# Banded attention in narrow query tiles: 32 local or 54 strided queries by 64 keys, stacked in the partitions, both heads in one transpose

## What is computed

```python
# 1: attention; heads 0-3 local, heads 4-7 strided
mask_local   = (rel >= 0) & (rel < 32)              # rel = query - key
mask_strided = (rel >= 0) & (key % 32 == query % 32)
attn = softmax(where(mask, q @ k.T / 8, -1e9)) @ v
# 2: x = attn (heads side by side, 512 wide)
theta = x @ w_theta
y = w_tok_r @ (x * cos(theta)) + w_tok_i @ (x * sin(theta))
u = x + y
x = u + relu(u @ w_ch)
# 3: four causal attention experts over x, top 2 of 4 by a gate, summed
```

## Time and profile before

| | us |
|---|---|
| median of 3 runs (584.88 to 585.02) | 584.98 |
| profiled execution, its own time | 586.84 |
| its span in the trace | 585.0 |
| TensorE matmul busy | 548.8 (94%) |
| VectorE busy | 348.0 (59%) |
| ScalarE busy | 259.3 (44%) |
| GpSimd busy | 130.4 (22%) |

### The profile page before, as it was taken

How to read it: one execution, slowest core, us unless ns; L and a number is a source line. 1 busy time by engine, 2 the same in 40 slices (tenths; PEclk the granted TensorE clock), 3 DMA queues, 4 the chain that set the end, 5 groups by cost and what they waited for, 6 DMA issues and landing times.

```text
span 585.0 us, 11660 instructions
## 1 busy us (share of the span) xinstructions
PE 548.8 (94%) x4473; PEld 468.8 (80%) x4473; DVE 348.0 (59%) x831; ACT 259.3 (44%) x774; POOL 130.4 (22%) x131
## 2 busy tenths in 40 slices
PE   6999999999999999999999999999999999998786
PEld 5777889989766799898866799898876799996555
DVE  1677856676779513676788622576778723344561
ACT  2774743556435531545533551455543551114242
POOL 3650800021312250013221250012322060000110
PEclk9999999999999999999999999999999999999879
DMA  9732046310000115121000014221000010000002
GB/s 219 198 92 74 1 126 152 77 29 21 2 1 2 72 23 120 41 55 28 3 0 2 37 47 113 62 46 31 8 2 1 34 49 1 1 1 1 1 0 82
DMA packets 73413, 27.13 MB, mean 46 GB/s; under 512 B 68624, under 2 KB 68624, under 8 KB 73360
## 3 DMA queue, kind: packets, MB, share of 16 engines
q1 hardware_dynamic: 68848, 24.38, 16.4%
q10 hardware_dynamic: 4512, 2.02, 1.4%
HBM read 21.67 MB, written 4.72 MB: 45 GB/s over the span
## 4 chain that ended last, share of the span: by engine, by line
PE 73%; DVE 15%; ACT 7%; issue 3%; POOL 1%; DVEq 0%; POOLq 0%; ACTq 0%
PE acc L1248 32%; PE wide L1248 14%; PE turned L1417 4%; PE wide L1320 4%; PE wide L1341 3%; PE turned L1361 3%; PE turned L1374 3%; DVE xt L1080 2%; PE turned L1391 2%; PE turned L1459 2%; ACT probs L877 2%; PE turned L1281 2%; DVE probs L1054 1%; DVE nmax L1023 1%; PE wide L1305 1%
## 5 line engine op out<-in xcount | busy, mean ns | idle before, releaser
L789 POOL TENSOR_TENSOR probs<-probs,rec 96x768 f32<-96x768 f32 (+1 forms) x16 | 21.7, 1354 | 203.1 <-DVE rec L1038 203.1
L870 ACT ACTIVATE probs<-wide,nmax 96x128 f32<-96x128 f32 (+1 forms) x176 | 61.3, 368 | 8.9 <-DVE nmax L1019 8.8
L885 ACT ACTIVATE pt<-turned 128x384 f32<-128x384 f32 (+3 forms) x64 | 30.8, 480 | 72.9 <-PE turned L1374 36.7
L877 ACT ACTIVATE probs<-wide,nmax 128x128 f32<-128x128 f32 (+4 forms) x72 | 39.0, 551 | 52.2 <-DVE nmax L1023 41.5
L798 POOL TENSOR_TENSOR probs<-probs,weight 128x128 f32<-128x128 f32 (+4 forms) x36 | 26.9, 767 | 155.6 <-DVE weight L1061 155.6
L1248 PE MATMUL wide<-w_tok_hi,z_hi 128*128 128x288 f32 x216 | 47.4, 300 | 0.0
L1248 PE MATMUL wide<-w_tok_hi,z_lo 128*128 128x288 f32 x216 | 46.0, 293 | 0.0
L1248 PE MATMUL wide<-w_tok_lo,z_hi 128*128 128x288 f32 x216 | 45.9, 293 | 0.0
L1023 DVE TENSOR_REDUCE nmax<-wide 128x1 f32<-128x128 f32 (+4 forms) x72 | 32.8, 512 | 16.9 <-PE wide L1346 16.9
L1248 PE MATMUL acc<-xu_hi,w_ch_hi 128*128 128x288 f32 x128 | 39.2, 306 | 2.0 <-DVE xu_lo L1150 2.0
L815 POOL TENSOR_TENSOR z_lo<-absf,z_hi 128x512 fp32r<-128x512 f32 x20 | 26.4, 1319 | 63.8 <-ACT z_hi L933 63.8
(11 more groups left out here) (190 smaller groups left out, 1479.5 us busy)
## 6 DMA issues: line engine op xcount, KB each, us to landing
raw_q<-in_q SPq DMA_DIRECT2D x32, 128.0 KB, 2.4
out<-o_sb SPq DMA_DIRECT2D x16, 256.0 KB, 2.0
raw_k<-in_k SPq DMA_DIRECT2D x28, 128.0 KB, 2.5
raw_v<-in_v SPq DMA_DIRECT2D x64, 31.5 KB
raw_v<-in_v SPq DMA_DIRECT2D x14, 120.0 KB
raw_r<-in_moe_w_tok_r SPq DMA_DIRECT2D x1, 1152.0 KB, 6.2
stage<-in_moe_w_theta ACTq DMA_DIRECT2D x2, 512.0 KB, 9.0
raw_i<-in_moe_w_tok_i SPq DMA_DIRECT2D x1, 1024.0 KB, 7.9
```

Of the source, the lines that this page charges most:

```text
L789: g.tensor_tensor(pr, pr, rec[0:rows, 1, 0:nt].unsqueeze(2).broadcast_to([rows, nt, w]), ALU.mult).then_inc(s["probs_pool"], 1)
L870: e = a.activation(probs[0:rows, hh, t * P:t * P + w], wide[slot][0:rows, t * P:t * P + w], ACT.Exp, bias=nmax[0:rows, hh, t:t + 1], accum ...
L877: e = a.activation(probs[:, hh, to0:to0 + n], wide[slot][:, at0:at0 + n], ACT.Exp, bias=nmax[:, hh, j:j + 1], accum_out=sums[:, hh, j:j + 1])
L885: ins = a.activation(dst, src, ACT.Copy)
```

## The change

The first attention gets smaller tiles, and several of them share a column of PSUM:

- A local tile is 32 queries by 64 keys (the 32 before and the tile's own 32), 18 per head. Four tiles stand above each other in the partitions, so a head has 5 columns of 64. A strided tile is 3 residues, 54 queries by 54 keys, 11 per head, two above each other, 6 columns.
- Both heads share one `wide` place, one bank each. The mask of a head is now one bf16 matmul (`copies_l` or `copies_s` by `mask_l` or `mask_s`), 320 or 384 wide, in place of three or two. One more small one per head (`never`) masks the keys before the first tile.
- The probabilities of the two heads lie side by side in `tiled` (head 0 in 64 columns, head 1 in the next 64), so one transpose turns both. `turn` is one step with 5 or 6 transposes in place of 12 or 10, and two copies in place of four. It waits for both heads: for VectorE's and for GpSimd's `norm`.
- `values` has one matmul for each small tile and head: 36 of 32 columns in place of 12 of 96, or 22 in place of 10. Its stationary operand is v, 64 columns wide as before, and head 1's rows are now 64 to 127.
- `max` reads 320 or 384 columns in place of 768 or 630, `exp` is 5 or 6 instructions per head of 64 columns in place of 6 or 5 of 128 or 126, and `norm` multiplies 320 or 384 columns.
- Order: between units of the first attention the scores come first and the whole turn after them. Before the third layer's first scores the whole turn comes first. In `LAST_PAIR` the turn comes behind three blocks of token weight transposes.
- Loads of v: a local pair's two heads lie in two halves of the partitions with the rows of v twice (6 DMAs as before, with 2304 rows of 256 bytes in place of 1472). A strided pair has 6 DMAs in place of 10.
- The constants are built in another order; the masks have a semaphore of their own (`masks`).

```diff
+W = 64
+L_T = S // STRIDE
+R_T = W // R_N
+COLS = (S_T * W + P - 1) // P
@@ attention_steps
+        if ahead and ahead[0] == "s1":
+            steps.append(("scores",) + ahead)
         if behind:
-            steps.append(("turn",) + behind + (0,))
+            steps.append(("turn",) + behind)
+        if ahead and ahead[0] != "s1":
+            steps.append(("scores",) + ahead)
         if ahead:
-            steps += [("scores",) + ahead, ("max",) + ahead + (0,)]
-        if behind:
-            steps.append(("turn",) + behind + (1,))
-        if ahead:
-            steps += [("max",) + ahead + (1,), ("exp",) + ahead + (0,)]
+            steps += [("max",) + ahead + (0,), ("max",) + ahead + (1,), ("exp",) + ahead + (0,)]
@@ LAST_PAIR
-LAST_PAIR = [("wtok", 0, "acc"), ("turn",) + S1_UNITS[-1] + (0,), ("wtok", NT, "wide"), ("wtok", 1, "wide"),
-             ("done", "wtok", 0, "acc"),
-             ("turn",) + S1_UNITS[-1] + (1,), ("values",) + S1_UNITS[-1], ("weights", 2),
+LAST_PAIR = [("wtok", 0, "acc"), ("wtok", NT, "wide"), ("wtok", 1, "wide"), ("done", "wtok", 0, "acc"),
+             ("turn",) + S1_UNITS[-1], ("values",) + S1_UNITS[-1], ("weights", 2),
@@ scores
+                    for hh in range(2):
+                        mm(wide[slot][:, hh * 512:hh * 512 + cols * W], copies[:, :],
+                           mask[:, :].unsqueeze(1).broadcast_to([part, cols, W]), start=True, stop=True,
+                           skip_group_check=True)
...
+                        row, at0 = part * t % P, part * t // P * W + (STRIDE if local(p) and t == 0 else 0)
+                        for hh in range(2):
                             hd = slice(hh * D, (hh + 1) * D)
+                            ins = mm(wide[slot][row:row + n, hh * 512 + at0:hh * 512 + at0 + q0 + n - k0],
+                                     qt[hd, q0:q0 + n], kt[hd, k0:q0 + n], start=False, stop=True,
+                                     skip_group_check=True)
@@ turn
+                            if n == 0:
+                                pe.wait_ge(s["probs_dve"], c.at("probs_dve"))
+                                pe.wait_ge(s["probs_pool"], c.at("probs_pool"))
+                            for t in range(ca, cb):
+                                k = min(P, part * nt - t * P)
+                                ins = nc.tensor.transpose(turned[slot][:, (t - ca) * P:(t - ca) * P + k],
+                                                          tiled[0:k, t, :], ident[0:k, 0:k])
@@ values
+                                ins = mm(turned[slot][hh * D:(hh + 1) * D, (t - ta) * rows:(t - ta) * rows + n],
+                                         raw_v[hh * W:hh * W + keys, p % 2, t, :],
+                                         tiled_t[hh * W:hh * W + keys, part * t:part * t + n], start=True, stop=True)
```

More of the change, by code:

```diff
@@ L178, in alone_steps @@
         nxt = units[i + 1] if i + 1 < len(units) else None
+        steps += early[i] + [("scores",) + ahead]
         if behind:
[L180 to L184, removed]
+            steps.append(("turn",) + behind)
+        steps += [("max",) + ahead + (0,), ("max",) + ahead + (1,), ("exp",) + ahead + (0,)]
         steps.append(("warm", 1 if nxt else 2, "acc", 1))
@@ L296, in psum_uses @@
     if k == "scores":
-        return ["wide"] * 2
+        return ["wide"] * (1 if step[1] == "s1" else 2)
     if k == "theta":
@@ L324, in events @@
         return {"negmax": 1}
+    if k == "exp" and step[1] == "s1" and step[4] == 0:
+        return {"exp_first": 1}
     if k == "norm":
@@ L533, in turned_copies @@
         def turned_copies(step, n, uses):
-            place, hh = turned[uses[n][0]], step[4]
+            place = turned[uses[n][0]]
             if step[1] == "s1":
-                rows, nt, w = tiles(step[2])
-                lo, hi = ((0, 3), (3, nt))[n]
-                return [(pt[0:w, hh, lo * rows:hi * rows], place[0:w, 0:(hi - lo) * rows])]
+                part, nt, _, cols = tiles(step[2])
+                lo, hi = ((0, 3 * P), (3 * P, nt * part))[n]
+                return [(tiled_t[:, lo:hi], place[:, 0:hi - lo])]
+            hh = step[4]
             blocks = turned_blocks(step[2], n, len(uses))
@@ L743, in after @@
                 step_n[0] += 1
[L745 removed]
+            for t, x in ((ident, 0.0), (ident_b, 0.0), (copies_l, 0.0), (copies_s, 0.0), (mask_l, 0.0), (mask_c, 0.0),
+                         (before, 0.0)):
                 after(g.memset(t[:], x))
+            after(g.memset(mask_s[:, 0:SQ], 0.0))
+            after(g.memset(mask_s[:, SQ:W], MASKED))
+            after(g.memset(never[:], MASKED))
             pool.wait_ge(s["const_step"], step_n[0])
@@ L878, in emit @@
                                              ACT.Exp, bias=nmax[:, hh, j:j + 1], accum_out=sums[:, hh, j:j + 1])
-                    e.then_inc(read["wide"][slot], 1)
+                    e.then_inc(s["exp_first"] if step[1] == "s1" and hh == 0 else read["wide"][slot], 1)
                 elif kind == "turn":
-                    note[("turned", step[4])] = uses[-1]
+                    for hh in step[4:] or range(2):
+                        note[("turned", hh)] = uses[-1]
                     for n in turned_by_scalar(step, len(uses)):
@@ L1297, in emit @@
                     p = step[2]
-                    rows, nt, w = tiles(p)
-                    slots = [free("wide", hh) for hh in range(2)]
-                    for slot in slots:
-                        for ta, tb in ((0, 1), (1, 4), (4, nt)) if local(p) else ((0, 4), (4, nt)):
-                            mask = mask_l[0:rows, min(ta, 1), :] if local(p) else mask_s[0:rows, :]
-                            mm(wide[slot][0:rows, ta * P:tb * P], ident_b[0:rows, 0:rows],
-                               mask.unsqueeze(1).broadcast_to([rows, tb - ta, P]),
-                               start=ta % 4 == 0, stop=True, skip_group_check=True)
+                    part, nt, rows, cols = tiles(p)
@@ L1319, in emit @@
+                    for t in range(nt):
+                        n = min(rows, S - rows * t)
+                        q0 = rows * t
+                        k0 = max(q0 - STRIDE, 0) if local(p) else q0
+                        row, at0 = part * t % P, part * t // P * W + (STRIDE if local(p) and t == 0 else 0)
+                        for hh in range(2):
                             hd = slice(hh * D, (hh + 1) * D)
-                            ins = mm(wide[slot][0:n, t * P:t * P + k1 - k0], qt[hd, rows * t:rows * t + n],
-                                     kt[hd, k0:k1], start=False, stop=True, skip_group_check=True)
```

221 lines of the change are left out of this document (104 added, 117 removed).

## The result

The changed kernel takes **596.7 us** (median; four runs from 595.2 to 599.8) against 585.0 us before: 2.1% slower, ratio 1.0208 with a 95% interval of 1.0171 to 1.0244. I had forecast 588.5 with a range of 580 to 594: the sign was right, the size was not. The profiled execution took 595.8 us, with a span of 594.0.

A forecast was written before the change was run, and what follows sets the result against it. TensorE, busy 94% of the span at nearly full clock, was taken as the bound. Three bodies +5.0 and prologue -1.3 made +3.7 on 586.84, 590.5 profiled and 588.5 by the median; whole range 580 to 594.

The forecast's parts named there:

- the new wait: Unit 3's turn ahead of the third layer's first scores: everything waits for GpSimd's norm, +1.95 us a body.
- Masks, turn: TensorE steps: local masks 0.75 to about 0.4 us; turn 1.0 to about 0.6 local, 0.62 strided.
- Local scores: TensorE, local unit: 72 records of 64 columns take 1.25 us plus 0.1 for never, against 1.43 before.
- Strided scores: TensorE, strided unit: 44 records with four tiles take 0.75 us, between 0.5 and 1.05, against 1.21 before.
- Local values: TensorE, local unit: 36 pairs paced by 64-wide weight loads take 2.2 us against 1.25, +0.95.
- Narrow values are cheap: Rival, 18%: a 32-column pair costs 0.027 to 0.03 us, local values take 1.2, the kernel 580.5 us, faster.
- Unit 3 ahead: Body, turn through turn: 2.85 becomes 2.2 us, -0.65, the turn waiting 0.4 to 0.6 for GpSimd's norm.
- The handover: Into the third layer: rank to next product 10.2 us against 8.24, TensorE idling some 2.7 us.
- The wait is short or given back: Rival, 22%: VectorE's chain starts earlier or the third layer's next wait absorbs the delay; 584 us, between 582.5 and 586.
- Prologue: Before the bodies: unit 0's turn ends earlier, theta starts about 44.7 instead of 45.99, -1.3 us, between -3 and +0.5.
- Tiles do not overlap: Rival, 8%: scores of neighbouring column groups go one after another, 597 us; about 605 if values collide in a bank.
- The sequencer binds: Rival, 2%: 62 ns a record adds 17 to 18 us a batch, about 650 us.

The follow-up runs named there:

- The two experiments: Changed kernel with third layer's first scores ahead of unit 3's turn, local values using half of v's columns (578.3 us) or half the query columns (584.6 us).
- the order experiment: Changed kernel with the third layer's first scores moved ahead of unit 3's turn: 583.5 us, ratio 0.9979 to the kernel before.
- half of v: Changed kernel with third layer's first scores ahead of unit 3's turn, and only 32 of v's 64 columns stationary in local values: 578.3 us.
- the shorter wait: Changed kernel with VectorE's gate chain moved behind norm of head 1 of unit 3: 587.1 us, ratio 1.0022 to the kernel before.
- the epilogue's fillers: Changed kernel with third layer's first scores ahead of unit 3's turn, plus filler matmuls in two waits of the epilogue's attention: 583.4 us.
- all together: Changed kernel with scores ahead of unit 3's turn, gate behind norm, fillers in two epilogue waits and three prologue waits: 581.0 us, ratio 0.9925.
- the filled wait: Changed kernel with five filler matmuls ahead of unit 3's turn in each body, the wait for GpSimd left: 593.8 us, ratio 1.0133.

## Why the prediction was wrong, and where it was right

**The step that failed** is the new wait: "Behind it wait the scores, their `max` and `exp`, and q and k products; nothing later gives it back." I priced an idle TensorE by the time it loses and let what comes behind run at the speed of the rows before. No term of the sum, and no rival, had a clock that falls. I had read that the clock is full in the bodies and had taken that as a property of the kernel, though it was one of a TensorE that never stood idle there. And the row to look at was in my own group: the two slices with a lower clock near the end are the half clock from 551.9 to 562.1, and it begins 1.7 us behind a wait of 1.94 us for `k` in the epilogue:

```profile
550.13 0.49 PE L1341 MATMUL wide<-k,q 64*128 64x128 f32 x4 [1.94 <-DVE k L1178]
```

With the filler in place the body costs 1.5 to 1.7 more, forecast 1.65; the fall of the clock adds 2.9, 1.5 and 1.5 us, 5.9 in all.

**Step by step.**
- *Masks, turn*: local masks 0.37, forecast 0.4, right. The turn took 0.78 for five transposes and 0.87 for six, forecast 0.6 and 0.62, too low.
- *Local scores*: 0.85 us, forecast 1.25, and `never` 0.02 in place of 0.1. Tiles in different column groups overlap more than I took; the lower bound of 0.5 held. Strided scores 0.70, forecast 0.75.
- *Local values*: 2.22, forecast 2.2, and for the reason given: weight loads. The two experiments show it. *Narrow values are cheap* falls.
- *Unit 3 ahead*: TensorE's wait for GpSimd at unit 2's turn was 0.59, forecast 0.4 to 0.6. Right; but with the longer turn the step took 2.66 from the masks at 137.92 to the next product at 140.58, forecast 2.2.
- *The handover*: wait 2.70, forecast 2.7; chain 10.2 with the idle time filled, forecast 10.2. Right without the clock. *The wait is short or given back* falls: it was given back nowhere.
- *Prologue*: theta started at 45.69, forecast 44.7, before 45.99: -0.3 in place of -1.3. In the changed kernel's trace TensorE waits 1.12 us for `kt` at unit 0, and from 17.6 to 21.0 it is granted 1.2 GHz; the turn takes 1.38 there in place of 0.83:

```profile
16.40 0.19 PE L1337 MATMUL wide<-never,ident_b 64*32 64x32 bf16 x2 [1.12 <-DVE kt L1031]
...
17.61 1.38 PE L1388 MATMUL turned<-ident,tiled 128*128 128x128 f32 x5 [0.29 <-POOL tiled L812]
```

  From that turn to unit 0's values it is 3.86 us, and 2.27 in the order experiment's trace, where the clock is full: 1.6 us for the same missing term. There theta started at 44.77, as forecast, but by luck. Unit 0's turn ended at 19.0, forecast 19.9, since GpSimd's scaling ended earlier in that execution, and the chain to the next turn's end took the 8.0 forecast. From there to theta it took 17.7 us, 0.9 more than before, where I had forecast 0.4 less. The 0.95 that unit 1's local values add was missing from the sum.
- *Tiles do not overlap* falls: 72 score records in 0.85 us are 12 ns each. The heads' values, rows 0 to 63 and 64 to 127 into one bank, keep the pace of the weight loads. With half of v they even overlap: at the pace of the prologue's fillers (16 records of 256 columns in 3.55 us) 72 records of 32 columns would need about 2.0 us one after another, an estimate, and they took 1.33. The Trainium skill's rule that different row tiles cannot access one PSUM bank at once (TensorEngine Tiling (Array Packing), Gotcha 1: PSUM Pressure) shows no cost here.
- *The sequencer binds* falls by the same row: 12 ns a record, 24 for each of the 36 matmuls. The Trainium skill's 62 ns for every matmul (TensorE: Matmul & The Clock Gate, Back-to-back issue gap) holds where hardware decode is off, by the page, and these rows are far below it.
- *From the profiled execution to the median*: I took off 1.86 us since the profiled run of before lay above its median. After the change the profiled run lies 0.9 below its median. That is 2.8 us of the error, and later runs of the kernel before had medians of 585.7 to 586.1, so the 584.98 was itself at the low end.

Added up: 590.5 was the forecast for the profiled execution, and 595.8 came: +5.6 in the bodies, +1.0 in the prologue, -1.3 in the epilogue. With the 2.8 of the last point that is the distance from 588.5 to 596.7. The rival that gave 597 (*tiles do not overlap*) had the right number for a reason that was wrong.

## What to carry to other kernels

Price a wait of TensorE twice: the time it stands, and the time after it, for the clock may be granted at half for some microseconds then; cutting a wait from 2.70 to 1.27 us here gave back two to three times the 1.4 us in each body. Whether a merged step now has to wait for the later of its two inputs is settled by the order around it: put the work that needs neither ahead of it, and the merging costs nothing. Where the stationary operand stays as wide while the moving one shrinks, the weight load sets the price.

## What the runs showed of the hardware that I had not expected

- After about 2.7 us of idle TensorE in a body that was otherwise full, the granted clock fell from 2.4 to 1.2 GHz in each of six cases (three bodies of the changed kernel, three of the old tiles with the whole turn ahead), for 3.4 or 6.8 us. After 1.27 us in the same place (the three bodies of the shorter wait) it did not, nor with the 2.7 us filled to 0.54. The fall came anywhere from 1.1 us before TensorE started again to 1.5 us after. Why it was followed by 3.4 us in some bodies and 6.8 in others stays open.
- A wait as short as 1.3 us is not safe elsewhere. In the prologue TensorE waited 1.12 to 1.61 us for `kt` ahead of unit 0's scores in four traces (the changed kernel, the shorter wait, the epilogue's fillers, all together), and its clock fell 0.4 to 1.5 us after that in all four; in the other nine it waited 0.6 us or less there and the clock did not fall. In the epilogue 3.4 us at half clock began 1.8 and 1.9 us behind a wait of 1.3 us for `k` in two traces (the filled wait, the old tiles with the whole turn). The length of a single wait does not decide it: in the filled wait's prologue 1.13 us of idle time at 18.0 was followed by no fall, and a fall at 43.8 came behind waits of 0.5 and 0.7 us.
- In the epilogue the same wait of 1.93 us for `k` was followed by half clock within 2 us in the order experiment (548.4 to 558.7), but not in the changed kernel, where the clock fell only later, at 567.1, 1.3 us behind another wait of 2.32 us. Which idle time lowers the clock there differs from trace to trace, and with it the time of the epilogue, from 81.4 to 84.9 us.
- Each us at half clock in which TensorE worked cost 0.43 to 0.46 us of a body's period, and 0.2 to 0.4 us of the epilogue's length, an estimate against the 80.7 us that the epilogue takes at full clock.
- Small fp32 matmuls in different row and column tiles go at 12 ns a record (72 in 0.85 us) where the columns that move are 64 and the stationary ones 32.
